# Storing the first quarter of the outputs: one point of issue, and another split over the DMA engines

## The reference, cut to what matters

```python
kv  = einsum('bhsd,bhse->bhde', k, v)         # 8 batches, 8 heads, 576 tokens, 64 wide
out = einsum('bhsd,bhde->bhse', q, kv)
out = out / sqrt(mean(out*out, -1) + 1e-6) * g_norm
x   = out as [4608 tokens, 512]
logits = x @ phi                              # 32 slots
d = softmax of logits over the tokens;  slot_input = d.T @ x
slot_out[e] = relu(slot_input[e] @ w1[e]) @ w2[e]      # 8 experts, 4 slots each
c = softmax of logits over the slots
return c @ slot_out                           # [4608, 512]
```

## Time and profile before

| | |
|---|---|
| time, median of three runs | 172.01 us |
| time of the profiled execution | 171.83 us |
| its span, first to last instruction | 170.5 us |
| bytes moved by DMA | 71.65 MB, mean 420 GB/s |
| PE busy | 149.9 us, 88% |
| time of the packets of SP's queue | 97.9% of 16 DMA engines' span |
| last output copy ends | 159.6 us |

### The profile page before, as it was taken

One profiled execution on the slowest core, in us unless ns is written; L12 is line 12 of the kernel. 1 busy time (PEld: TensorE's weight loads), 2 busy tenths in 40 slices (PEclk: granted clock), 3 DMA queues, 4 the chain that ended last, 5 costly groups with the idle time before them and its releaser, 6 DMA issues.

```text
span 170.5 us, 4242 instructions
## 1 busy us (share of the span) xinstructions
PE 149.9 (88%) x1836; PEld 104.4 (61%) x1836; DVE 86.8 (51%) x185; ACT 89.1 (52%) x230; POOL 59.7 (35%) x73
## 2 busy tenths in 40 slices
PE   7988897989999899999899998989999989989200
PEld 3467776979678888896697674346655533554000
DVE  1122156283677266762946698823888136318300
ACT  3036576796975986859759864202233044418300
POOL 7000707648357745377382679500000004000000
PEclk9999999999999999999999999999999999999755
DMA  5999999999999999989999999999999999999996
GB/s 184 420 423 432 426 430 429 482 416 435 484 410 408 458 428 415 434 384 467 400 465 392 459 409 407 450 429 415 430 427 446 452 434 392 414 422 443 411 455 288
DMA packets 4365, 71.65 MB, mean 420 GB/s; under 512 B 790, under 2 KB 790, under 8 KB 922
## 3 DMA queue, kind: packets, MB, share of 16 engines
q1 hardware_dynamic: 3994, 71.18, 97.9%
q0 software_dynamic: 352, 0.20, 0.4%
HBM read 61.94 MB, written 9.44 MB: 419 GB/s over the span
## 4 chain that ended last, share of the span: by engine, by line
PE 59%; DMA 13%; ACT 12%; DVE 6%; SPq 2%; issue 1%
PE psum L215 59%; DMA arena<-in_kv_dram 13%; ACT bd L215 3%; ACT sq L215 3%; ACT xall L215 2%; SPq L215 2%; DVE logits L215 1%; DVE ms L215 1%; ACT part L215 1%; ACT arena L215 1%; ACT d L215 1%; DVE part L215 1%; ACT r L215 1%; DVE acc L215 1%; DVE r L215 0%
## 5 line engine op out<-in xcount | busy, mean ns | idle before, releaser
L215 PE MATMUL psum<-bd,arena 128*128 128x192 f32 (+1 forms) x320 | 56.1, 335 | 2.0 <-ACT bd L215 1.6
L215 PEld LDWEIGHTS psum<-bd,arena 128*128 128x128 f32 (+1 forms) x320 | 45.4, 179 | 8.7 <-ACT bd L215 2.9
L215 DVE TENSOR_REDUCE ms<-sq 128x16 f32<-128x1024 f32 (+1 forms) x19 | 22.1, 1162 | 32.5 <-ACT sq L215 32.2
L215 POOL TENSOR_TENSOR part<-part,r 128x512 f32<-128x512 f32 x17 | 17.8, 1049 | 49.5 <-DVE r L215 49.5
L215 POOL TENSOR_TENSOR xall<-xall,r 128x512 f32<-128x512 f32 x34 | 34.8, 1043 | 0.0
L215 ACT ACTIVATE sq<-psum 128x512 f32<-128x512 f32 x36 | 21.5, 598 | 12.3 <-PE psum L215 12.1
L215 PEld LDWEIGHTS psum<-arena 128*64 128x64 f32 (+1 forms) x640 | 19.0, 137 | 8.1 <-DMA arena<-in_kv_dram 3.3
L215 PE MATMUL psum<-arena 128*64 128x64 f32 (+1 forms) x640 | 21.7, 226 | 2.1 <-DMA arena<-in_kv_dram 2.0
L215 ACT COPY xall<-psum 128x512 f32<-128x512 f32 x34 | 20.6, 606 | 0.0
L215 ACT COPY part<-psum 128x256 f32<-128x256 f32 (+1 forms) x38 | 13.6, 359 | 8.8 <-DVE part L215 7.6
L215 DVE TENSOR_REDUCE logits<-part 128x64 f32<-128x512 f32 (+1 forms) x18 | 17.9, 992 | 0.0
(11 more groups left out here) (80 smaller groups left out, 126.8 us busy)
## 6 DMA issues: line engine op xcount, KB each, us to landing
arena<-in_w_dram SPq DMA_DIRECT2D x4, 4096.0 KB, 23.5
arena<-in_w_dram SPq DMA_DIRECT2D x4, 2048.0 KB, 20.0
arena<-in_t_dram SPq DMA_DIRECT2D x1, 6912.0 KB, 36.0
arena<-in_w_dram SPq DMA_DIRECT2D x2, 3072.0 KB, 22.7
arena<-in_kv_dram SPq DMA_DIRECT2D x2, 2304.0 KB, 23.4
arena<-in_kv_dram SPq DMA_DIRECT2D x1, 4608.0 KB, 42.6
arena<-in_kv_dram SPq DMA_DIRECT2D x1, 3584.0 KB, 32.2
arena<-in_kv_dram SPq DMA_DIRECT2D x3, 1152.0 KB, 13.4
```

Of the source, the lines that this page charges most:

```text
L215: inst = getattr(engine, method)(*args, **kwargs)
```

## The change

The first group now leaves behind chunk 2 in one go. In the few words that come with the change: "Chunks 0 to 2 stored behind chunk 2: GpSimd moves odd rows to engines 0 to 6, 7 and 8, and 15 with one step between; SP the even part in two transfers." The engines of that sentence are DMA engines.

GpSimd gets three entries: 14 partitions (1, 5, ... 53) with all three chunks, 18 KB a row, a = 7; 14 partitions (73, 77, ... 125) with chunks 0 and 1, 12 KB a row, a = 2; then the step of 6; then 4 partitions (57 to 69) with all three chunks, a = 3 and c = 3. SP gets four: the 64 even partitions, 18 KB a row; the 32 partitions 3, 7, ... 127, 18 KB a row; and chunk 2 of the 14 partitions from 73 on, in an entry of nine rows (a = 3) and one of five rows (a = 2, c = 2). The step of 7 ahead of the experts is gone.

```diff
 FIRST = (
-    ("sync", 1, 4, 30, 5, 1, 0, 1), ("sync", 121, 4, 2, 3, 3, 0, 1),
-    ("gpsimd", 1, 4, 24, 2, 1, 1, 2), ("gpsimd", 97, 4, 8, 2, 1, 1, 2),
-    ("sync", 3, 4, 32, 1, 1, 0, 2), ("sync", 0, 2, 64, 1, 1, 0, 3), ("sync", 1, 2, 64, 1, 1, 2, 3),
+    ("gpsimd", 1, 4, 14, 7, 1, 0, 3), ("gpsimd", 73, 4, 14, 2, 1, 0, 2), ("gpsimd", 57, 4, 4, 3, 3, 0, 3),
+    ("sync", 0, 2, 64, 1, 1, 0, 3), ("sync", 3, 4, 32, 1, 1, 0, 3),
+    ("sync", 73, 4, 9, 3, 1, 2, 3), ("sync", 109, 4, 5, 2, 2, 2, 3),
 )
-STEPS = (7, 6)
+STEPS = {1: 6}
...
-    steps = list(STEPS[::-1])
-
-    def store_first(n):
+    def store_first():
         at = 0
-        for engine, p0, step, m, a, c, k0, k1 in FIRST:
+        for i, (engine, p0, step, m, a, c, k0, k1) in enumerate(FIRST):
             size = (k1 - k0) * CHUNK
...
+            getattr(nc, engine).dma_start(dst, src)
+            if i in STEPS:
+                step_over(STEPS[i])
             at += m * size
...
-        if n <= OUT_ROWS[0][-1]:
-            store_first(n)
+        if n == OUT_ROWS[0][-1]:
+            store_first()
...
-    step_over(steps.pop())
     expert_h(0)
```

More of the change, by code:

```diff
@@ L927, in step_over @@
         nc.gpsimd.dma_start(*ends)
-    steps = list(STEPS[::-1])
-    def store_first(n):
+    def store_first():
         at = 0
-        for engine, p0, step, m, a, c, k0, k1 in FIRST:
+        for i, (engine, p0, step, m, a, c, k0, k1) in enumerate(FIRST):
             size = (k1 - k0) * CHUNK
[L935 to L942, removed]
-                    step_over(steps.pop())
+            src = place(OUT_AT[k0], size)[p0 : p0 + step * (m - 1) + 1 : step]
+            dst = out[:, at : at + m * size]
+            if c > 1:
+                src = src.rearrange("p (c n) -> p c n", c=c)
+            dst = dst.rearrange("o (b a n) -> (o a) b n", a=a, n=size // c)
+            getattr(nc, engine).dma_start(dst, src)
+            if i in STEPS:
+                step_over(STEPS[i])
             at += m * size
```

## The result

The changed kernel took 173.55 us (median of six runs, 173.35 to 173.85) beside 172.0 us (171.83 to 172.06) for the kernel before on the same chip: 1.0097 times as long, 95% interval 1.0087 to 1.0108. The forecast was 172.0 in a range up to 172.6, so it was wrong by 1.5 us. The profiled execution took 173.35 us, its span is 172.0 us.

The account below looks back on a forecast made before the run. It took bytes over 16 DMA engines as the bound, the last engine setting the end. Last packet -0.1 to +0.25 us against 170.1, taken as 0, other parts 0: 172.01 + 0 = 172.0 us, range 171.45 to 172.6.

Parts of the forecast that it names:

- 5 and 6, the light middle ones, from 168.55 to 169.5: End of DMA engines 5 and 6, read as light middle ones: 24 KB more each, +0.91 us, ending at 169.5.
- or from 169.35 to 170.3 if the unexplained loss was theirs and comes again: Alternative end of engines 5 and 6, if the one engine's unexplained loss of about 1 us was theirs: 170.3.
- the experts and chunk 11 keep their times: Last load: GpSimd's two 18 KB packets add 1.4 us on middle engines, 148.85, no later than the late five at 148.9.
- 0, 7 and 8 stay where they are, up to 170.0: End of engines 0, 7 and 8: bytes unchanged, so their ends stay, up to 170.0 us.
- at best like SP's rows (0), at worst shared over other engines: GpSimd's untried 18 KB rows and one-engine transfer: 0 if like SP's rows; sharing over other engines was left to a rival.
- The prediction's last line: Signs of a wrong forecast: fetches fall on other engines than before, or GpSimd's 18 KB packets run slower than SP's.
- theory P: Follow-up theory, not in the prediction: which SBUF rows (partitions) the DMA engines read is what stretches packets.
- the key of engines: Entries' split: a pieces go to a engines, SP's from engine 0, GpSimd's from its last stop; held to some 0.5 us.
- The lone end that I had named as its sign: Sign of the rival that engine 15 is not early (172.6 us, chance 0.10): one end 0.5 us behind the rest.
- the rule on engines 7 and 15: Trainium skill's rule, speaking against the change: engines 7 and 15 usually slower than the rest; these carry most here.
- Levelled: Rival: 1 and 2 light, the loss not repeated, 0, 7 and 8 gain: up to 0.55 us, 171.46 to 171.65; chance 0.17.
- Runs dry: Rival: SP's first store ready only at 147.0, engines 0, 7, 8 idle 1.0 us: 172.9; chance 0.07 together with pieces elsewhere.

Follow-up runs that it names:

- Plain: Changed kernel with the first group as one SP transfer of 128 rows of 18 KB behind chunk 2, nothing by GpSimd, no step: 172.5 us, 1.0032.
- halves: Changed kernel with the first group as two SP transfers of 64 neighbouring rows of 18 KB, nothing by GpSimd: 177.5 us, 1.0324.
- evens: Changed kernel with the first group as two SP transfers of 64 rows, one of even rows, one of odd, nothing by GpSimd: 172.58 us, 1.0040.
- the exchanged rows: Changed kernel with the rows of GpSimd's first two entries swapped, SP's two small entries moved with them, same bytes per engine: 173.55 us, 1.0095.
- the four neighbouring ones: Probe on the changed kernel: SP moves rows 16 to 127 as one transfer, GpSimd rows 0 to 3 and 4 to 7 in 6 KB packets: 174.37 us, 1.0152.

## Why the prediction was wrong

**The sum that came out.** Two steps failed, and one of them set the time. Packets that stretch moved the last end from 170.1 to 171.65: that is the whole way from 172.0 to 173.55. The other, 24 KB more on late engines, is hidden behind it: 5 and 6 end at 170.65. Plain, with the same KB on them and without the stretch, puts it at 0.5 us.

**"5 and 6, the light middle ones, from 168.55 to 169.5": failed.** I had the earlier trace rows as counts only and gave the classes to engines as fitted best. 5 and 6 belong to the five that stood at 144.0, as the kernel with their 72 KB shows in its profiled run. By the prediction's own terms they then end at 169.85 + 0.91 = 170.76; two engines ended at 170.63 and 170.67. The look-out beside it, "or from 169.35 to 170.3 if the unexplained loss was theirs and comes again", was nearer but for the wrong reason.

**"the experts and chunk 11 keep their times": failed by the same step.** It allowed 1.4 us of GpSimd's packets among the load rows of a middle engine. On late ones, 148.9 + 1.4 = 150.3, and PE's wait ends at 150.51. Chunk 11 is 1.11 us late by that. It costs next to nothing: the engines that stand idle around 161.2 to 161.6, some 0.55 us in sum, are those that end first.

**"0, 7 and 8 stay where they are, up to 170.0": failed, and set the time.** Their bytes are unchanged, but the packets are not. The step bounded GpSimd's 18 KB rows by "at best like SP's rows (0), at worst shared over other engines". A third case was missing: packets of both queues took longer than their size asks for, 6.3 engine-us more than before. One of 7 and 8 lost 1.86 us in seven GpSimd packets, the other nothing; engine 0, the only one with 3 KB packets, lost 0.58 us in these. The mean end of the 16 engines moved from 169.57 to 170.04, and 6.3 / 16 = 0.39 of that 0.47 is stretch. The prediction's last line names 18 KB packets of GpSimd that run slower as a sign of being wrong, but gives it no price: three of these 14 did (0.85, 0.96 and 1.61 us), and cutting them to 6 KB did not help the time.

What stretches them is shown in part. That the rows read can do it is shown by halves against evens. That the uneven reading by GpSimd's and SP's small entries does it in the changed kernel is argued, not shown: without these entries the stretch is 1.3; the later issue and a dry queue don't explain it, long rows at most a part (5.6 and 6.4 in place of 7.9), and another order of the entries makes it larger. Against it stand two forecasts of theory P that missed, the exchanged rows and the four neighbouring ones. No run altered only the rows of these entries and took the stretch away.

**Right:** the key of engines (5 and 6 in the kernel with their 72 KB; 2.74 us for 72 KB). Engine 15 did not set the end: its twelve 6 KB packets from GpSimd lost 0.2 us, and the packets that abut behind them lead to ends between 169.56 and 171.03. The lone end that I had named as its sign came, 0.43 us behind the next, but it fits 7 or 8. Which of these two, the trace does not tell, so the rule on engines 7 and 15 stays open. The step was worth 0 where it stood. The lag of GpSimd's transfers held: first packet at 147.72, 3.9 us behind the issue at 143.79; I had put that issue 0.7 us too early. SP's four issues took 3.39 us instead of 2.4 to 2.9, with no effect, as the share was 1.04 from 145 to 150.

**The rivals.** Levelled fell, since one of 7 and 8 lost instead of gaining. "Runs dry", priced at 172.9, came nearest in time, but the runs don't bear out its mechanism: the share at 146 to 147 us is 0.95 (0.98 before), and filling SP's queue earlier left the stretch at 7.8. The chance of 0.21 for slower had no case in it for the true mechanism.

## What to carry to other kernels

Where DMA bounds, read bytes and busy share together: a share at 1.0 with fewer GB/s meant here that packets stretched, and then a table of KB per engine no longer gives the ends. Cut a store so that each transfer reaches over all partitions evenly (172.5 us against 177.5), and give extra bytes only to engines whose own end has been identified: send one of them a large piece and see which end moves, in more than one run. A count of ends without names isn't enough.

## What the runs showed that I had not expected

- Same bytes, same packets, other partitions: 172.5 against 177.5 us, with 18 KB packets that took up to 2.9 us instead of 0.686.
- Packets of the other queue need not stretch with a transfer: GpSimd's 24 packets on rows 0 to 7 kept their 234 ns while SP's 18 KB packets took up to 2.29 us. On rows 0, 4, 8, 12 and 1, 5, 9, 13 they did stretch; why, no run shows.
- Engines with little to do can't be emptied early: in the kernel with 72 KB moved off 7 and 8, five engines ended within 0.13 us of each other, at 168.74 to 168.87, as they had waited for the last store.
- An entry of seven rows from GpSimd seems to move the place of the next one in another way than an entry of 14 rows cut in seven. The Trainium skill (DMA: Bandwidth & Descriptors, "Why a DMA increments its semaphore by 16 and not by 1") knows an exception for some of GpSimd's direct copies, which are spread as if over all 16. The two lone ends at 173.97 and 174.43 would fit it, but no run shows which engines they are.
- One kernel had two times 1.5 us apart (172.9 and 174.45) in four runs. The two times fit the two readings of 5 and 6, late or middle, so the classes of the engines may change from run to run; no run settled it.

Open: why the old table, whose odd rows are uneven too, stretches by only 1.6 us, and how much of the changed kernel's 6.3 us each entry brings. No run here beats the kernel before; by the earlier trace rows a better split of the same bytes could give 0.55 us at most.
